# Second MLP of an attention and two-MLP kernel: the input product in Strassen's form, seven products for eight

## The reference, cut to what matters

```python
def _moe_ref(x, w_gate, w_val, w_out):        # first MLP, 512 -> 1536 -> 512
    gate = 1.0 / (1.0 + np.exp(-(x @ w_gate)))
    val = x @ w_val
    return (gate * val @ w_out).astype(np.float32)

def _moe2_ref(x, w_in, w_out):                # second MLP, 512 -> 2048 -> 512
    h = x @ w_in
    relu6 = np.clip(h + 3.0, 0.0, 6.0)
    g = h * relu6 / 6.0
    return (g @ w_out).astype(np.float32)

def reference(**kwargs):
    attn_out = _attn_ref(**attn_kwargs)       # 4 batches, 8 heads, 576 positions, head size 64
    x = attn_out.transpose(0, 2, 1, 3).reshape(B * S, H * D)     # 2304 tokens x 512
    x = _moe_ref(x=x, **moe_kwargs)
    return _moe2_ref(x=x, **moe2_kwargs)
```

## Time and profile before

| | us |
|---|---|
| median of 3 runs | 1111.74 |
| lowest and highest run | 1111.37, 1111.90 |
| the profiled execution, its own time | 1112.64 |
| its span, first to last instruction | 1110.8 |

### The profile page before, as it was taken

One profiled execution on the slowest core, in us unless ns is written; L12 is line 12 of the kernel. 1 busy time (PEld: TensorE's weight loads), 2 busy tenths in 40 slices (PEclk: granted clock), 3 DMA queues, 4 the chain that ended last, 5 costly groups with the idle time before them and its releaser, 6 DMA issues.

```text
span 1110.8 us, 20581 instructions
## 1 busy us (share of the span) xinstructions
PE 1091.7 (98%) x6928; PEld 1016.9 (92%) x6928; DVE 581.1 (52%) x1308; ACT 558.8 (50%) x1258; POOL 501.0 (45%) x519
## 2 busy tenths in 40 slices
PE   5999999999999999999999999999999999999998
PEld 4668999999999999999999999999999999899997
DVE  5897766767766767766733333633223232322322
ACT  5777676677676677776654333223223232232322
POOL 5887567568567568667535445992000000000000
PEclk9999999999999999999999999999999999999999
DMA  7553333433433433432212323340000000000000
GB/s 183 130 132 76 105 104 95 108 104 91 115 103 93 110 104 83 122 105 72 79 56 80 82 79 103 116 131 31 7 0 28 0 28 0 0 28 0 29 1 29
DMA packets 100248, 81.68 MB, mean 74 GB/s; under 512 B 7760, under 2 KB 85584, under 8 KB 100176
## 3 DMA queue, kind: packets, MB, share of 16 engines
q1 hardware_dynamic: 100176, 80.77, 26.9%
HBM read 76.03 MB, written 4.72 MB: 73 GB/s over the span
## 4 chain that ended last, share of the span: by engine, by line
PE 94%; DVE 2%; DMA 1%; ACT 1%; issue 1%; SPq 0%; POOL 0%; DVEq 0%; ACTq 0%
PE ps L613 88%; PE ps L654 4%; PE ps L668 1%; DMA stage<-w_val 1%; DVE prob L1243 0%; DMA qk_st<-qk_t 0%; DVE q_s L1159 0%; SPq L360 0%; DVE pt_lo L1191 0%; ACT h_gate L1100 0%; ACT WG L970 0%; DVE Y L1389 0%; DVE znorm L1213 0%; DVE znorm_e L1215 0%; ACT x_hi L1011 0%
## 5 line engine op out<-in xcount | busy, mean ns | idle before, releaser
L613 PE MATMUL ps<-x_hi,WG 128*128 128x288 f32 x1536 | 323.8, 297 | 1.1 <-DVE pt_lo L1191 0.6
L613 PEld LDWEIGHTS ps<-x_hi,WG 128*128 128x128 f32 x1536 | 251.3, 188 | 3.6 <-issue 1.2
L613 PE MATMUL ps<-x_lo,WG 128*128 128x288 f32 x768 | 226.1, 294 | 0.0
L613 PE MATMUL ps<-c_hi,W 128*128 128x384 f32 x768 | 210.3, 337 | 0.0
L523 POOL TENSOR_TENSOR WG<-stage,WG 128x512 fp32r<-128x512 f32 x96 | 128.0, 1350 | 115.6 <-ACT WG L970 115.4
L613 PE MATMUL ps<-W,g_hi 128*128 128x512 f32 x576 | 179.0, 391 | 0.0
L1411 DVE SCALAR_TENSOR_TENSOR g_raw<-g_raw,ps 128x384 f32<-128x384 f32 x96 | 53.1, 554 | 219.2 <-ACT g_raw L1132 219.2
L613 PE MATMUL ps<-h_hi,WO 128*128 128x288 f32 x768 | 164.5, 297 | 0.2 <-DVE Y L1389 0.2
L1132 ACT ACTIVATE g_raw<-ps 128x384 f32<-128x384 f32 x96 | 47.3, 492 | 214.4 <-PE ps L613 214.3
L543 POOL TENSOR_SCALAR prob<-prob,rscale 128x128 f32<-128x128 f32 (+4 forms) x160 | 110.4, 708 | 78.6 <-DVE rscale L1203 78.6
L613 PEld LDWEIGHTS ps<-x_lo,WG 128*128 128x128 f32 x768 | 144.2, 188 | 0.5
(11 more groups left out here) (107 smaller groups left out, 1850.6 us busy)
## 6 DMA issues: line engine op xcount, KB each, us to landing
stage<-w_out SPq DMA_DIRECT2D x64, 256.0 KB, 2.7
qk_st<-qk_t SPq DMA_DIRECT2D x54, 288.0 KB, 4.1
stage<-w_gate SPq DMA_DIRECT2D x48, 256.0 KB, 3.3
stage<-w_val SPq DMA_DIRECT2D x48, 256.0 KB, 3.1
qn_st<-q_n SPq DMA_DIRECT2D x16, 256.0 KB, 3.2
stage<-w_in SPq DMA_DIRECT2D x16, 256.0 KB, 2.7
out<-y_out SPq DMA_DIRECT2D x5, 768.0 KB, 3.5
v_st<-v_n SPq DMA_DIRECT2D x12, 256.0 KB, 2.7
```

Source lines behind the costliest of these rows:

```text
L613: return pe.matmul(o, l, r, start=start, stop=stop, skip_group_check=True)
```

## The change

Only the second MLP's input product changes its form, and what feeds it. A chunk is now 768 tokens, seen as two halves of 384, the 512 input features as two halves of 256, and a pair of hidden tiles (2 x 128 features) as two columns. The product of a 2 x 2 block weight matrix with a 2 x 2 block input is formed by Strassen's scheme: seven products of sums in place of eight plain ones. Each product is 2 x 3 matmuls of 384 columns into one of two PSUM banks (6 and 7), and is added, with its sign, into one or two of four SBUF tiles `Cb`. Relu, multiplication and the cut into high and low follow from there. There are 24 steps (three chunks, eight pairs of hidden tiles). The output product of step s - 1 is issued in single units between the products of step s, into banks 0 to 5.

The weights of the seven products (five sums, two plain blocks, each in high and low part, 1.8 MB a pair) are made beside the last four quarters of the first MLP, one pair of hidden tiles for each half quarter: two 256 KB loads on SP, five sums on VectorE (`prep_sums`), three high copies on ScalarE (`prep_hi`), three low subtractions on GpSimd (`prep_lo`), one write to DRAM (`write_parts`). In the second MLP each step's weights are read back from DRAM, product by product, two steps ahead. The inputs' sums are made by VectorE for the first chunk (`first_sums`) and by GpSimd for the others; their high and low parts by `x_high2` and `x_lower2`. The outputs leave PSUM into the part of Y that is no longer needed, and go to DRAM from there. GpSimd cuts only the output weights now. The loops over quarters and chunks are written out.

```diff
 @@ walk
-            quarter(n_pairs - QPB, 0)
-            with eng.Fori(1, QPB - 1) as q:
-                quarter(q + (n_pairs - QPB), q)
-            quarter(n_pairs - 1, QPB - 1)
+            for q in range(QPB):
+                quarter(n_pairs - QPB + q, q)
 @@ sync
+            def load_raw_in(e):
+                for i in two:
+                    f = pair_of_f(e, i)
+                    sp.dma_start(raw_in[e % 2][i][:, :].rearrange("p (k c) -> p k c", c=P),
+                                 by_row_tile(w_in)[:, :, f * P:(f + 1) * P]).then_inc(p_ld[e % 2], DMA)
+            def write_parts(e):
+                sp.wait_ge(p_lo, 3 * (e + 1))
+                sp.dma_start(parts[e, :, :], WC[e % 2][:, :, :, :].rearrange("p a b c -> p (a b c)").bitcast(F32)).then_inc(p_wr[e % 2], DMA)
...
+                    for x, (ahead, k) in enumerate([x for slot in CUT[p] for x in slot]):
+                        if prep is not None and prep >= 1 and x == 1:
+                            write_parts(prep - 1)
+                            if prep + 1 < FP:
+                                load_raw_in(prep + 1)
...
+                for i in range(PROD) if s + 2 < n_steps else ():
+                    sp.wait_ge(c_prod, PROD * s + i + 1)
+                    at = STORE[i] * 4 * P
+                    sp.dma_start(WC[s % 2][:, STORE[i], :, :].rearrange("p b c -> p (b c)").bitcast(F32),
+                                 parts[pair_at(s + 2), :, at:at + 4 * P]).then_inc(c_ld[s % 2], DMA)
 @@ gpsimd
+            def prep_lo(e):
+                j = e % 2
+                pool.wait_ge(p_hi, 3 * (e + 1))
+                for at, src in ((slice(0, 5), AS[j][:, :, :]), (slice(5, 6), raw_in[j][0][:, 0:2 * P].unsqueeze(1)),
+                                (slice(6, 7), raw_in[j][1][:, 2 * P:4 * P].unsqueeze(1))):
+                    pool.tensor_tensor(WC[j][:, at, 1, :], src, WC[j][:, at, 0, :].bitcast(F32), ALU.subtract).then_inc(p_lo, 1)
...
                 low_ws(r, p, cut)
+                if not (scoring or old):
+                    prep_lo(prepared(r, p))
 @@ tensor
+            def product(s, i):
...
+                if g < 2:
+                    pe.wait_ge(f_y, OU * (n_pairs + 1) - 1 + g)
+                else:
+                    s0, i0 = divmod(g - 2, PROD)
+                    if i0 < 2:
+                        pe.wait_ge(c_copy, 4 * s0 + 2 + i0)
+                    else:
+                        pe.wait_ge(c_add, 8 * s0 + (2, 4, 6, 7, 8)[i0 - 2])
+                for k in two:
+                    w = [WC[j][:, STORE[i], part, k * P:(k + 1) * P] for part in two]
+                    last = hi_lo(prod_bank(s, i), w, XC[i][:, 0, k, :], XC[i][:, 1, k, :], k == 0, k == 1)
+                last.then_inc(c_prod, 1)
...
+            for s in range(n_steps + 1):
+                x = 0
+                for i, several in enumerate((2, 2, 2, 2, 2, 1, 1)):
+                    if s < n_steps:
+                        product(s, i)
+                    for x in range(x, x + several) if s else ():
+                        out2_unit(s - 1, x)
+                    x += 1
 @@ scalar
+                    if alone and i == 1 and prepared(r, p) == FP - 1:
+                        for x in range(PROD):
+                            x_high2(0, x)
+                    if alone and i == 2 - p:
+                        prep_hi(prepared(r, p))
 @@ vector
+            def x_lower2(c, i):
+                dve.wait_ge(xs_hi, PROD * c + i + 1)
+                dve.tensor_tensor(XC[i][:, 1, :, :], x_source(c, i), XC[i][:, 0, :, :].bitcast(F32), ALU.subtract).then_inc(xs_lo, 1)
+            def prep_sums(e):
+                j = e % 2
+                dve.wait_ge(p_ld[j], 2 * DMA * (e // 2 + 1))
...
+                dve.tensor_tensor(AS[j][:, 0, :], a11, a12, ALU.add).then_inc(p_sum, 1)
...
                 for i in range(QT):
+                    if alone and i == 1 - p:
+                        e = prepared(r, p)
+                        prep_sums(e)
+                        first_sums({0: (0, 1), 2: (2, 3), 4: (4,)}.get(e, ()))
...
                             j = int(unit[1])
-                            if j == 0 and not has_next_quarter(r):
-                                cut_chunk(0)
+                            for x in {0: (0, 1, 2), 2: (3,), 4: (4,), 6: (5,), 7: (6,)}.get(j, ()) if not has_next_quarter(r) else ():
+                                x_lower2(0, x)
...
+                added(s, 3, 1, 4, 0)
+                added(s, 3, 2, 4, 0)
+                g_low(s, 0)
+                if next_x:
+                    x_lower2(c + 1, 0)
+                    x_lower2(c + 1, 1)
+                times_relu(s, 1)
+                added(s, 4, 2, 4, 4)
+                added(s, 4, 3, 4, 2)
+                g_low(s, 1)
+                if next_x:
+                    x_lower2(c + 1, 2)
+                added(s, 5, 2, 4, 5)
+                if next_x:
+                    x_lower2(c + 1, 3)
+                times_relu(s, 2)
+                added(s, 6, 3, 4, 6)
+                if next_x:
+                    x_lower2(c + 1, 4)
```

More of the change, by code:

```diff
@@ L450, in _ @@
             n = n_pairs * BLK
[L451 to L458, removed]
@@ L459, in _, with load_out2 @@
-            for t in range(CT):
[L460 to L466, removed]
+            def load_out2(x):
+                f = used[x]
+                staged(n + x, (n + x) % NST, w_out2[f * P:(f + 1) * P, :], False)
@@ new lines, in _, with store @@
+            for x in range(NST):
+                load_out2(x)
+            write_parts(FP - 1)
+            def store(c, tiles):
+                at = 2 * CH * c
+                rows = slice(at + tiles[0] * P, at + (tiles[-1] + 1) * P)
+                sp.wait_ge(o_left, CT * c + tiles[-1] + 1)
+                if tiles[0] < DT:
+                    src = Y[:, tiles[0]:tiles[-1] + 1, at:at + BANK]
+                    sp.dma_start(out[rows, :].rearrange("(t p) c -> p t c", p=P), src).then_inc(stored, DMA)
+                else:
+                    sp.dma_start(out[rows, :].rearrange("p (a c) -> p a c", a=2), out_place(c, tiles[0])).then_inc(stored, DMA)
@@ L1138, in store2, with copied @@
[L1138 to L1150 removed]
+            def copied(s, i, y, scale):
+                act.wait_ge(c_prod, PROD * s + i + 1)
+                if s >= 1:
+                    act.wait_ge(c_mul, 4 * (s - 1) + y + 1)
+                act.activation(Cb[y][:, :], prod_bank(s, i), ACT.Copy, scale=scale).then_inc(c_copy, 1)
@@ L1153, in _ @@
+            g_high(n_steps - 1, 3)
+            for t in range(CT):
+                leave(n_steps // FP - 1, t)
         @block.vector
@@ L1416, in _, with added @@
-            products2(0)
-            with dve.Fori(1, n_chunks) as n:
-                cut_chunk(n)
-                products2(n)
-            dve.wait_ge(b_st, DMA * n_chunks)
-            dve.wait_ge(b_end, 1)
-            dve.tensor_copy(y_out[:, 0, :], ps[:, 4, :]).then_inc(b_first, 1)
+            def added(s, i, y, before, after):
+                dve.wait_ge(c_prod, PROD * s + i + 1)
+                dve.wait_ge(c_copy, 4 * s + before)
+                if after:
+                    dve.wait_ge(c_add, 8 * s + after)
+                dve.tensor_tensor(Cb[y][:, :], prod_bank(s, i), Cb[y][:, :], ALU.add).then_inc(c_add, 1)
@@ L1425 @@
+            g_low(n_steps - 1, 2)
+            times_relu(n_steps - 1, 3)
+            g_low(n_steps - 1, 3)
 def kernel(**inputs):
```

337 lines of the change are left out of this document (230 added, 107 removed).

## The result

The changed kernel takes 1124.4 us (median of 4 runs, 1120.71 to 1126.88), the kernel before 1111.82 beside it on the same chip (1111.37 to 1112.42). The ratio is 1.011, 95% interval 1.0082 to 1.0139: slower by 1.1%, 8.4 us above the forecast of 1116 and inside its range. Its runs differ by 6 us, those of the kernel before by 1.

A forecast was written before the change was run, and what follows sets the result against it. TensorE (PE), busy for 1091.7 of 1110.8 us, was taken as the bound. 1112.6 - 25.3 + 15.4 + 4.0 + 3.4 + 6.8 = 1116.9, with the median 0.9 lower: 1116 us, range 1097 to 1127.

The forecast's parts named there:

- What is removed: Second MLP's input product: 144 fewer matmuls at 0.176 us over 24 steps, -25.3 us; steady step 15.7 us.
- the reload was never late: Rival for the second MLP: weight reloads from DRAM come late, 1 us in 22 steps, 1138 us; chance 0.05.
- The preparation: Quarters 12 to 14: VectorE's sums, held by GpSimd's long subtraction, delay V3's low half; 4.4 + 5.5 + 5.5 = +15.4 us.
- The write: Quarters 13 and 14: 1.8 MB write, 4.9 us, queued ahead of a weight load, shifts subtraction and sums by 1.1 us.
- the order: VectorE's queue in quarters 12 to 14: sums ahead of V4 and V3's low half, a stall of 4.4 us each.
- the prep does not hold PE: Rival at V3's low half in the quarters: sums are over in time, no stall, 1096 us; chance 0.15.
- PE slows after its waits: Rival: each of five waits of 4 to 5.5 us is followed by a slow stretch costing 2.5 us, 1128; chance 0.10.
- Handover: Between the MLPs: the first product waits for Y's seventh evacuation behind VectorE's six x_lower2, +4.0 us.
- turns: Chunk changes at steps 7/8 and 15/16: x_lower2 and GpSimd's sums delay products, 3.4 us a turn, +6.8 us.
- Step 0: Second MLP's first step: the copy and add chain runs without output units between, 10.8 us against 7.4, +3.4 us.
- The median: Whole kernel: median of the runs taken as 0.9 us below the profiled execution, so 1116 from 1116.9.

The follow-up runs named there:

- e1: Changed kernel with VectorE's five weight sums behind the value units V4 and V5 in the second half of each lone quarter; 1115.38 us, ratio 1.0035.
- e3: Changed kernel with VectorE's sums behind V5 and the 1.8 MB write issued later, behind raw loads and gate blocks; 1106.05 us, ratio 0.9951.
- e8: e3 with 3, 6 and 10 idle VectorE copies ahead of V4's low half in quarters 12, 13, 14; 1118.52 us (one run).
- e5: e3 with two X low parts moved behind Y's last evacuation, and GpSimd's last preparation waiting for them in 14 short pieces; 1101.27 us, ratio 0.9914.
- e2: Changed kernel with GpSimd's three low-part subtractions cut into 14 of 128 columns, VectorE's order unchanged; 1118.09 us, ratio 1.0068.
- e6: e5 with GpSimd's X sums in halves of 384 columns and a third buffer; 1097.25 us, ratio 0.9881.
- e7: e6 with the seven products of step 0 in seven PSUM banks instead of two; 1096.98 us, ratio 0.9876.
- e9: e7 with GpSimd's preparation of pair 7 in seven subtractions of 256 columns, without their wait for VectorE's low parts; 1098.88 us, ratio 0.9889.
- e10: Changed kernel with only the 1.8 MB write issued three SP issues later, VectorE's sums left in place; 1118.33 us, ratio 1.0067.

## Why the prediction came out as it did

- **What is removed** was right: the steady step is 15.69 us without a PE wait, for 15.7 forecast, and the reload was never late (256 KB in 2.7 us). That rival is out. The saving was 24.3 us and not 25.3: the old step took 16.70 us, where 15.7 and six matmuls of 0.176 make 16.8; most distances of 384 columns are 0.174.
- **The preparation** was right in mechanism and place. GpSimd's subtraction began 15.5 us into quarter 12 and the sums 15.75; the forecast had 15.7 and 15.8. The waits are 13.6 us, 1.8 less than the 15.4: the five sums were over in 5.6 us, not 6.3. The write took longer than I had it (7.4 us for 4.9); quarter 13 waited 5.1 us for the forecast's 5.5 all the same. I had given the write 1.1 us a quarter on top of the order; it put 1.6 on the waits, and by itself, in e1, it makes waits of 3.7 and 3.4. The rival *the prep does not hold PE* is out, and e3 shows what it was worth: the sums only had to stand behind V5 and the write behind the gate blocks.
- **PE slows after its waits** is where the sum failed. I gave it 0.10 as a rival, as if it either happened or not; it belonged in the sum. In the quarters it took 5.9 us (20.3 less 13.6 of waits and 0.8 of restarts), and e8 shows that it follows from the wait alone. At the handover the first four products ran at 7.0 us for 4.2, but the step is held by its chain too: at a clock of 1.00 step 0 still took 10.0 us in e5 and 11.0 in e2, for 12.5. So the fall was worth 1.5 to 2.5 of the 5.1 there; these kernels differ in other ways too, and a closer figure is open. I had asked for 2.5 us behind each of five waits; it came behind four, at 1.5 to 2.6. My reason against it, that no row of before shows a fall, was true of the only wait there, which came while PE was slow anyway. The granted clock of 1.00 that the forecast read at 8 to 12 us stands against a matmul of 0.45 us, so it is not to be taken for full clock; in the changed kernel's trace the stretch from 16 to 22 us, with such matmuls, reads 0.50.
- **Handover** 3.1 for 4.0 and **turns** 6.65 for 6.8: right in size. GpSimd's long instruction in the middle of VectorE's queue is 1.7 us of the handover (e2); e6 took 4.0 us from the turns with shorter pieces and one more buffer together. **Step 0**'s chain was right (e6, e7, e9): 2.6 to 3.6 us at full clock for the 3.4 forecast, the rest is the clock.
- The sum with what was measured: 1112.6 - 24.3 + 20.3 + 3.1 + 5.1 + 6.65 - 2.8 = 1120.7, for 1120.71 profiled. The 2.8 are the first 590 us, which the change doesn't touch. That the profiled execution lies only 3.8 us above the 1116.9 is in part luck: the quarters cost 4.9 us more than forecast, step 0 1.7 more, and the saving was 1.0 smaller; the early start took 2.8 us off, the handover and the turns 1.0.
- **The median** lies 3.7 above the profiled execution; I had taken it 0.9 below. There is one trace, so what the others lost is open. Two hints: quarter 12 begins at 590.70 us in this trace and between 591.3 and 592.9 in those of the eleven experiments, so this execution was 0.6 to 2.2 us ahead of the others. And the PE wait of 1.9 us at a turn was followed by a fall of the clock in four of sixteen cases (both turns of e1, the second of e3, 0.63 from 969 to 973, and of e5). The step then took 19.4 us for 17.8 or 17.9, so 1.5 us more; in the changed kernel's trace neither turn had it. It was not shown that either happened in those runs, and their mean granted clocks, 0.989 to 0.991, are not below the 0.988 of the profiled one.

## What to carry over

Before an engine that is half idle gets more work, ask what stands behind the new instructions in its queue and who waits for that: five operations of 0.4 us, one place too early, cost 4.6 us a quarter, and moved by one slot, with the write out of the way too, no more than the 0.6 that is left. Two causes of one wait hide each other: remove both before you judge either. Where GpSimd and VectorE both read SBUF with two operands, the length of GpSimd's single instruction is the price of meeting it, so keep it short or place it where VectorE has none. Waits of PE as long as those here (3 to 5 us) are to be priced at their length and about half as much again; waits of about 1 us each (e6) cost their length and a restart of some 0.3. Splitting alone is not enough: two waits of 1.67 and 2.02 us close together (e1) were followed by half clock as well.

## What the runs showed of the hardware

- Each of the 25 PE waits of 1.94 us and more from quarter 12 on, in all traces with the change, was joined or followed by a stretch at a granted clock of 0.50 (in the quarters 1.5 to 2.6 us lost). Of the 16 waits of 1.88 to 1.93 at the turns four were (1.5 us each), and of those of 1.8 and less that stood alone none.
- Each PE wait costs some 0.3 us beyond its length at full clock (0.26 in the quarters, 0.2 to 0.35 at the turns): the end of the matmul before it and a slower first one.
- A two-operand VectorE operation of 256 columns took 0.41 us alone, 0.68 beside pieces of 128 columns, 0.94 beside pieces of 256, 3.18 beside one of 1280.
- 256 KB that was issued behind the 1.8 MB write landed after 7.8 us (raw loads, median), and issued ahead of it after 4.0 (e10); other blocks alone after some 3.
